# Linear attention, gated MLP and mixture of experts on one core: scores of two tiles in a row, the state faded by ScalarE, three token differences after attention

## The reference

```python
for b in range(nb):                       # blocks of 64 tokens
    intra = einsum('bhic,bhjc->bhij', qb, kb) * Dmask      # decayed scores within the block
    intra = einsum('bhij,bhjd->bhid', intra, vb)
    inter = einsum('bhid,bhde->bhie', qb * lam_pow, kv_state)
    out[:, :, sl] = intra + inter
    kv_state = lam_block * kv_state + einsum('bhsd,bhse->bhde', kb * rev_pow, vb)
x = attention output as (1536, 512)
x = (silu(x @ w_gate) * (x @ w_val)) @ w_out               # w_gate, w_val: 512 x 1536
out[mask] = gate_w * (relu(x[mask] @ w1[e]) @ w2[e])       # the one expert of each token
```

## Time and profile before

| | us |
|---|---|
| median of 3 runs (lowest, highest) | 535.84 (535.03, 536.0) |
| profiled execution, its own time | 536.05 |
| its span, first to last instruction | 534.3 |
| TensorE busy in it | 525.4 |
| VectorE, ScalarE, GpSimd busy | 353.3, 247.1, 74.4 |
| attention on TensorE, first `scores` to first `gate_val` | 5.75 to 48.37 |

### The profile page before, as it was taken

How to read it: one execution, slowest core, us unless ns; L and a number is a source line. 1 busy time by engine, 2 the same in 40 slices (tenths; PEclk the granted TensorE clock), 3 DMA queues, 4 the chain that set the end, 5 groups by cost and what they waited for, 6 DMA issues and landing times.

```text
span 534.3 us, 8608 instructions
## 1 busy us (share of the span) xinstructions
PE 525.4 (98%) x3275; PEld 447.9 (84%) x3275; DVE 353.3 (66%) x609; ACT 247.1 (46%) x414; POOL 74.4 (14%) x94
## 2 busy tenths in 40 slices
PE   8999999999999999999999999999999999999995
PEld 7998888888888887887888888778999999999994
DVE  7889898796775647644556666567667666766620
ACT  4325464635354425442434544465555565555511
POOL 4991000000000000010000020023021130311001
PEclk9999999999999999999999999999999999999999
DMA  8997304213030305645244666267575656654001
GB/s 291 339 302 255 137 21 158 104 54 126 32 120 20 119 0 176 187 158 230 81 138 133 203 196 237 81 212 238 210 272 204 206 221 215 220 201 169 1 28 36
DMA packets 22281, 84.57 MB, mean 158 GB/s; under 512 B 3804, under 2 KB 3804, under 8 KB 18656
## 3 DMA queue, kind: packets, MB, share of 16 engines
q1 hardware_dynamic: 17376, 71.35, 39.0%
q0 software_dynamic: 3712, 10.54, 5.6%
q10 hardware_dynamic: 1152, 2.13, 1.0%
HBM read 75.59 MB, written 10.53 MB: 161 GB/s over the span
## 4 chain that ended last, share of the span: by engine, by line
PE 95%; issue 2%; DVE 1%; POOL 1%; POOLq 0%; ACT 0%
PE bank L934 18%; PE bank L859 16%; PE bank L1161 15%; PE bank L1171 12%; PE bank L867 12%; PE bank L891 6%; PE bank L1075 2%; PE bank L1094 2%; PE bank L783 2%; PE bank L821 1%; PE bank L794 1%; PE bank L1150 1%; PE bank L829 1%; PE bank L961 1%; PE bank L1204 1%
## 5 line engine op out<-in xcount | busy, mean ns | idle before, releaser
L1609 DVE TENSOR_TENSOR ewl<-stages,ewh 128x1024 fp32r<-128x1024 f32 x50 | 60.8, 1223 | 16.9 <-ACT ewh L1248 16.6
L1248 ACT ACTIVATE ewh<-stages 128x1024 fp32r<-128x1024 f32 x50 | 52.2, 1054 | 0.7 <-DMA stages<-expert_w 0.7
L1554 ACT ACTIVATE ehh<-bank 128x256 fp32r<-128x256 f32 x48 | 18.5, 385 | 58.1 <-PE bank L1161 58.0
L636 POOL DMA_DIRECT2D stages<-expert_w x8 | 4.6, 572 | 260.9 <-DVE more_hl L1609 185.3
L1171 PE MATMUL bank<-ewl,ehh 128*128 128x512 f32 x96 | 37.8, 394 | 0.0
L1171 PE MATMUL bank<-ewh,ehl 128*128 128x512 f32 x96 | 37.7, 393 | 0.0
L1171 PE MATMUL bank<-ewh,ehh 128*128 128x512 f32 x96 | 37.5, 391 | 0.0
L1161 PEld LDWEIGHTS bank<-exh,ewh 128*128 128x128 f32 x224 | 33.2, 188 | 3.6
L1161 PE MATMUL bank<-exh,ewh 128*128 128x256 f32 x224 | 36.0, 283 | 0.0
L2092 DVE SCALAR_TENSOR_TENSOR ehl<-bank,ehh 128x256 fp32r<-128x256 f32 x48 | 20.2, 422 | 23.8 <-ACT ehh L1554 23.7
L1161 PE MATMUL bank<-exl,ewh 128*128 128x256 f32 x224 | 34.9, 278 | 0.0
(11 more groups left out here) (291 smaller groups left out, 1248.6 us busy)
## 6 DMA issues: line engine op xcount, KB each, us to landing
stages<-expert_w SPq DMA_DIRECT2D x21, 1024.0 KB, 4.9
stages<-mlp_w SPq DMA_DIRECT2D x24, 768.0 KB, 4.5
stages<-attn_in SPq DMA_DIRECT2D x18, 512.0 KB, 5.6
stage<-expert_w SPq DMA_DIRECT2D x7, 1024.0 KB
stages<-expert_w POOLq DMA_DIRECT2D x8, 512.0 KB, 5.7
stage<-attn_in SPq DMA_DIRECT2D x6, 512.0 KB, 5.8
held<-c SPq DMA_DIRECT2D x12, 256.0 KB, 2.0
stages<-held SPq DMA_DIRECT2D x12, 256.0 KB, 2.8
```

The source lines that it names most:

```text
L1248: return nc.scalar.activation(dst, src, ACT.Copy)
L1554: nc.scalar.activation(ehh[f % 2][:, :], bank[:, H_BANK + f % 2, 0:CAP], ACT.Relu).then_inc(ehh_ready, 1)
L1609: V.tensor_tensor(dst, src, high.bitcast(F32), ALU.subtract).then_inc(inc, 1)
```

## The change

Five edits. (1) From n = 5 on, TensorE runs scores only in the odd tiles, and then for the two tiles n+1 and n+2 in a row: pairs 6 and 7, 8 and 9, 10 and 11. (2) `fade` moves from GpSimd to ScalarE, as four activations of 128x128 behind the output copies of tile n-2. (3) GpSimd runs `queries(n)` before `keys(n)`. (4) The router's small transfer is issued behind all tiles' instead of behind tile 0's. (5) On VectorE `add_state(0)` moves behind `weigh(1)`; of the four differences `turn(1, t)` that stood between the last tiles only the first stays there, and three go behind attention; the output weights' low parts and those of the second gate and value weights go further back, between the steps of the plain units.

```diff
+PAIRED = 5
@@ sync
             for s in range(4):
                 attention_in(s, s)
-                if s == 0:
-                    sp.dma_start(router[:, :, 0:E], router_w).then_inc(router_landed, 16)
             for n in range(4, NT):
                 sp.wait_ge(o_ready, n - 3)
                 attention_in(n % 4, n)
+            sp.dma_start(router[:, :, 0:E], router_w).then_inc(router_landed, 16)
@@ gpsimd
-            def fade(n):
-                pool.wait_ge(state_ready, 2 * (n - 1))
-                nc.gpsimd.tensor_tensor(faded[n % 2][:, :, :], state[n % 2][:, :, :],
-                                        powers[:, H:H + NPAIR, P:P + 1].broadcast_to([P, NPAIR, P]),
-                                        ALU.mult).then_inc(faded_ready, 1)
-
             for n in range(1, NT):
+                if n >= 2:
+                    queries(n)
                 if n < LAST_STATE:
                     keys(n)
-                if n >= 2:
-                    queries(n)
-                if 2 <= n < LAST_STATE:
-                    fade(n)
@@ tensor
-                if 1 <= n < NT - 1:
-                    scores(n + 1)
+                for m in (n + 1,) if 1 <= n < PAIRED else (n + 1, n + 2) if n >= PAIRED and n % 2 else ():
+                    if m < NT:
+                        scores(m)
                 within(n)
@@ scalar
+            act.wait_ge(pair_step, 8)
+
+            def fade(n):
+                act.wait_ge(state_ready, 2 * (n - 1))
+                for a in range(NPAIR):
+                    last = nc.scalar.activation(faded[n % 2][:, a, :], state[n % 2][:, a, :], ACT.Copy,
+                                                scale=powers[:, H + a, P:P + 1])
+                last.then_inc(faded_ready, 1)
+
             for n in range(NT):
                 attention_tile(n)
+                if n + 2 < LAST_STATE:
+                    fade(n + 2)
@@ vector
                 weigh(n)
                 if n == NT - 1:
                     split_gate_val(0, 0)
+                if n == 1:
+                    add_state(0)
                 if n >= 1:
                     tokens_low(n - 1)
-                if n < LAST_STATE:
+                if 1 <= n < LAST_STATE:
                     add_state(n)
-                if n >= NT - 4:
-                    turn(1, n - (NT - 4))
-            split_out(0, 0)
+                if n == NT - 4:
+                    turn(1, 0)
             tokens_low(NT - 1)
-            split_mlp(0, 1)
...
+            for t in range(1, 3):
+                turn(1, t)
             start_gate(0, 0)
+            turn(1, 3)
+            split_gate_val(0, 1)
+            start_hidden(0, 0)
             for t in range(2):
                 turn(0, t)
-            start_hidden(0, 0)
+            split_out(0, 0)
+            start_low(0)
+            start_gate(1, 0)
             for t in range(2, 4):
                 turn(0, t)
-            start_low(0)
-            start_gate(1, 0)
             split_turn(T1)
             start_hidden(1, 0)
+            split_out(0, 1)
             sum_weights(1, range(3))
             start_gate(0, 1)
```

## The result

| us | before | changed |
|---|---|---|
| median of 8 runs each, on one chip (lowest, highest) | 535.96 (535.03, 536.42) | 536.94 (536.31, 538.0) |
| profiled execution, its own time | 536.05 | 536.81 |
| its span | 534.3 | 534.9 |

What follows compares the result with a forecast made beforehand. TensorE, busy 525.4 of 534.3 us, was taken as the bound, so out_product(0,0)'s start decides: -1.05 - 0.50 - 0.9 + 0.2 + 0.15 + 0.55 + 0.5 = -1.05, predicting 534.8 us, range 533.6 to 536.6.

Steps and rivals of the forecast that it cites:

- what comes back in attention: Attention's last tiles: new waits give back 0.2 (transfers), 0.15 (`pt` of tile 11) and 0.55 us (first weights).
- the first weights: Ahead of gate_val(0,0): weights landing in 5.3 us, then `gvh` and `gvl`, make TensorE wait 0.55 us; bounds 0 and 1.0.
- Scores in a row: TensorE in attention: three visits to scores fall away at 0.35 us each, minus 1.05 us; bounds 0 and 1.05.
- Queries before keys: GpSimd, tile 2: `qs` is ready earlier, so from_state(2) no longer waits; minus 0.50 us.
- The turn: VectorE, last tiles: the token differences no longer collide with GpSimd's queries(10), removing waits; minus 0.9 us.
- Router last: Transfer queue at the start: gives the first tiles a little lead, for which nobody waits any more; no cost counted.
- scores(9) and (11): TensorE in attention: landings of 4.5 us against 4.44 available, a wait of 0.1 at each, 0.2 in all; bounds 0 and 2.3.
- Rival C: Attention: at 5.6 us of landing scores(9) and scores(11) wait 1.15 each; +1.1, 536.9 us; chance 0.12.
- `pt` of tile 11: Attention: weigh(11) waits for tokens_low(9), so `pt` comes about 0.15 us after TensorE wants it.
- The plain units: Behind attention: VectorE's third `sg` comes late, so TensorE waits 0.5 us ahead of gate_val(1,1); bounds 0 and 1.3.
- "slower": Whole kernel: slower than before by more than 0.2%, given a chance of 0.11.
- the Trainium skill's rule: VectorE turn against GpSimd queries: whoever starts first wins; the forecast said the trace agrees on blocking, not on the winner.

Runs made afterwards that it cites:

- number 2: The changed kernel with the router's transfer back behind tile 0's: 536.36 us, 1.0006 of the kernel before.
- number 4: The changed kernel with VectorE's old order from the last four tiles on: 536.48 us, 1.0015 of the kernel before.
- number 5: The changed kernel with 10 instead of 8 dummy matmuls ahead of scores(0): 536.73 us, 1.0018 of the kernel before.
- number 7: number 2 with the last turn and the second `gvl` ahead of the first `sig` on VectorE: 535.17 us, 0.9995 of the kernel before.
- number 12: The kernel before with the paired scores alone: 536.24 us, 1.0012 of the kernel before.
- number 10: number 7 plus the early requests of number 6, without paired scores: 534.94 us, 0.998 of the kernel before; with pairs 534.16.
- number 3: The changed kernel without pairs, one scores group a tile throughout: 537.99 us, 1.0035 of the kernel before.
- number 11: number 7 plus the early requests of number 6, with the router's transfer last: 534.66 us, 0.9982 of the kernel before.
- number 1: The kernel before with the router's transfer issued behind all tiles': 536.78 against 535.68 us, ratio 1.0013.
- number 6: number 2 with each half, and the first weights, asked for as soon as their own place is free: 534.82 us, 0.9986 of the kernel before.
- number 9: The kernel before with 6 instead of 8 dummy matmuls ahead of scores(0): 535.99 us, 1.0008 of the kernel before.

## Why the prediction was wrong

The step that failed is the one on transfers, "what comes back in attention": with "I take 4.5, a wait of 0.1 at each", and for the first weights "So 0.55". Tile 9's first half was there 5.3 us after its issue (34.94 - 29.64), not 4.5, and those of tiles 8 and 10 took 6.0; only tile 11's met the forecast (asked for at 37.16, no wait at 41.60). I had taken the late landing of 4.7 for the rule, and the median of 5.6 for that of second halves and of the first burst. And the first weights, now issued 1.85 us behind tile 11's second half, took 6.4 us.

Which place waits is partly a matter of the execution. In six profiles the kernel has the pairs and SyncE's old rule (the changed one, numbers 2, 4, 5, 7 and 12). Tile 9's first half took 5.3 in the first and 3.8 to 4.0 in the other five, where scores(9) waits for no transfer; in number 5 scores(7) waits 0.51 in its place. So 4.5 at scores(9) was not far off, but rested on one landing where there was a spread. What failed in all six is the weights: 6.4 to 7.3 us, where the forecast had 5.3 and 0.65 for the queue. In the four of them in which VectorE is not later still, gate_val(0,0) waits 0.81 to 1.27 instead of 0.55 (spacing from within(11) less 0.96). Why a landing takes 4 or 6 us the runs don't show.

Point by point, in the profiled executions:

- **Scores in a row**, -1.05: 1.00 from start to start at (6)-(7) and (10)-(11); worth 0.97 by number 10. Right.
- **Queries before keys**, -0.50: 1.42 became 0.92. Right.
- **The turn**, -0.9: 0.69 long. Right, but with luck: it started at 39.42, queries(10) had ended at 39.33. In numbers 3, 5 and 11, with the same order, the two met and the turn took 1.15, 0.92 and 0.80.
- **Router last**, costed at nothing: +0.24 at `to_state(0)`; 0.5 to 0.6 us in the median by numbers 2 and 11 and 1.1 by number 1, the only one of the three differences that is clear of its interval, with a tail by the late clock. Landings late in attention are long with the router first too (6.6 in number 2), so the rest of its price has no place of its own. Wrong: I weighed who waits for the router, not what stands in the queue in its place.
- **scores(9) and (11)**, +0.2: 0.86 and 0. Short by 0.66. Rival C's mechanism, at one of its two places, and in this profile alone.
- **The first weights**, +0.55: 0.81, short by 0.26. Their landing of 6.4 had been put at 5.3 plus 0.65 for the queue.
- **`pt` of tile 11**, +0.15: 0.26.
- **The plain units**, +0.5: 0.73, of it 0.5 at the predicted place, the gate half of gate_val(1,1). The mechanism is shown by number 7, which took 0.65 of it away by moving two steps ahead of the first `sig`.

The errors add to 0.24 + 0.66 + 0.26 + 0.11 + 0.23 = 1.50; out_product(0,0) came 0.60 later instead of 1.05 earlier, 1.65 apart, and 0.15 stays spread over steps of a few hundredths. The sign came from the sum of five terms that all erred to the same side. The remaining 0.4 us, between 0.60 in the spans and 0.98 in the medians, is not in one profile: 0.12 is time outside the span (1.87 instead of 1.75), the profiled execution lies 0.13 below its median, and that of the kernel before 0.09 above its own. Rival C had the right size (536.9 by 1.15 at each scores) with a chance of 0.12; the wait was smaller than C's, and the router and the units made up the sum. On the whole "slower" had 0.11 and should have had more, since C was priced by a median that I argued away.

## What to carry to other kernels

When work is moved forward on an engine that hardly ever rests, list for each moved group every input it waits for and put the slack beside it, with the whole spread of landings of that stretch and not the best one; here 4.4 us of slack met landings of 3.8 to 5.3 for tiles 9 and 11. If the slack is short, ask for data when its own place is free, not when the whole slot is. And a transfer that nobody waits for still holds a place in the queue: moving it changes who lands when.

## What the runs showed of the hardware

- **A small transfer's place.** The router's weights, issued behind tile 0's, went with a first landing of 4.1 to 4.4 us after issue in the kernels that have it there, and 4.6 to 5.1 in those that have it last (eight profiles and six). In those with the router last, SyncE issues tile 1's first half at 2.2 instead of 2.9 us. How that delays a transfer issued before it was not tried further.
- **Late rise of TensorE's pace.** The granted clock is 1.00 in all these rows, so the levels are read from the matmuls' spacing. Six executions had TensorE idle for 0.56 us or more ahead of scores(0). In four (idle 0.56, 0.58, 0.84, 0.85) the matmuls kept the 1.2 GHz pace up to some 10.5 us; in two (0.69 each, the changed kernel and number 11) they had 2.4 GHz at once. Without such a gap the full pace came between 4.9 and 7.1 us. So idle time there risks 1.5 to 1.9 us at the start, and its length alone doesn't decide; what else does stays open. Once the full pace had come, idle time of 0.73 ahead of scores(1) (number 6) did not end it.
- **The turn on VectorE and queries on GpSimd shut each other out, and the first one wins.** In eight profiles the turn at tile 8 overlapped a queries operation (queries(10), in number 1 queries(9)), and in each it ended 0.54 or 0.55 us after it, whatever its own start (lengths from 0.80 to 1.75). In number 2 the turn started 0.07 us ahead, took its 0.69, and queries(10) took 1.66:

```profile
38.15 0.69 DVE L1745 TENSOR_TENSOR xt<-xt 128x512 f32<-128x512 f32 x1
```

```profile
38.22 1.66 POOL L602 TENSOR_TENSOR qs<-stages,powers 128x512 f32<-128x512 f32 x1 [2.28 <-DMA stages<-attn_in]
```

  So the Trainium skill's rule, SBUF — State Buffer, section "SBUF: two separate sides", first come first served, agrees with these rows, where I had said that the trace speaks against it: in the earlier trace rows the two starts are 0.02 us apart, too close for the record to tell who was first.
- **A landing goes with what was issued just before.** The first weights took 5.1 and 5.3 us to land in the two profiles in which they were issued 3.1 us behind tile 11's second half with nothing between (number 9, before), and 6.4 to 7.3 in the six in which that gap was 1.85 us (in three of them with the router's transfer in it). In numbers 1 and 3 the gap was 3.1 us with the router's transfer in it, and they took 5.8 and 6.7, so the gap is not all of it, and no run moved it alone. An earlier issue can gain less than it moves: number 2 issued them 1.27 us before the changed kernel did (38.11 against 39.38), and `gvh`, which waits for them, started 0.39 us earlier.
